# Nine small per-partition tables take 64 B instead of 256 B each, and the buffers behind them move in SBUF

## What is computed

```
qn = q / (norm(q, axis=rows) + 1e-6);  kn likewise
a  = softmax(kn^T @ qn / tau)                 # 256 x 256
x  = v @ a                                    # 6016 x 256
h  = x @ w_in1;  g = h - tanh(h);  x2 = g @ w_out1
h2 = x2 @ w_in2; g2 = where(h2 > 0, h2, exp(min(h2, 0)) - 1)
out = g2 @ w_out2
```

## Time and profile before

| | us |
|---|---|
| median of 3 runs (lowest to highest) | 1094.74 (1094.33 to 1095.83) |
| the profiled execution's own time | 1094.33 |
| its span, first to last instruction | 1092.5 |
| PE busy | 1083.3 (99%) |
| PEld busy | 907.8 (83%) |
| DVE busy | 708.0 (65%) |
| ACT busy | 536.1 (49%) |

### The profile page before, as it was taken

One profiled execution on the slowest core, in us unless ns is written; L12 is line 12 of the kernel. 1 busy time (PEld: TensorE's weight loads), 2 busy tenths in 40 slices (PEclk: granted clock), 3 DMA queues, 4 the chain that ended last, 5 costly groups with the idle time before them and its releaser, 6 DMA issues.

```text
span 1092.5 us, 14169 instructions
## 1 busy us (share of the span) xinstructions
PE 1083.3 (99%) x4908; PEld 907.8 (83%) x4908; DVE 708.0 (65%) x1139; ACT 536.1 (49%) x893; POOL 0.8 (0%) x7
## 2 busy tenths in 40 slices
PE   8999999999999999999999999999999999999998
PEld 7887888888888888888888888888888888888898
DVE  5886666666665766666666666666576666666565
ACT  6675545444444544544544544444454454444443
POOL 0000000000000000000000000000000000000000
PEclk9999999999999999999999999999999999999999
DMA  9941010110100101101011011010010010000010
GB/s 355 324 120 20 1 20 0 20 20 1 20 6 15 20 0 19 19 0 19 0 19 19 0 19 19 0 19 13 6 19 0 14 19 0 0 14 7 1 20 15
DMA packets 106237, 33.42 MB, mean 31 GB/s; under 512 B 96864, under 2 KB 101344, under 8 KB 105952
## 3 DMA queue, kind: packets, MB, share of 16 engines
q1 hardware_dynamic: 105776, 32.13, 11.7%
q10 hardware_dynamic: 432, 0.92, 0.2%
HBM read 26.87 MB, written 6.16 MB: 30 GB/s over the span
## 4 chain that ended last, share of the span: by engine, by line
PE 97%; DVE 1%; ACT 0%; DMA 0%; issue 0%; ACTq 0%
PE h_ps L375 15%; PE h_ps L377 15%; PE h_ps L376 15%; PE x_ps L375 8%; PE x_ps L376 8%; PE x_ps L377 8%; PE out_ps L375 8%; PE out_ps L376 8%; PE out_ps L377 8%; PE x_ps L383 4%; DMA q_ring<-q_dram 0%; DVE g_lo L710 0%; DVE wf_lo L740 0%; DVE w_out_lo L710 0%; DVE g L845 0%; ACT g_hi L651 0%
## 5 line engine op out<-in xcount | busy, mean ns | idle before, releaser
L710 DVE TENSOR_TENSOR g_lo<-g,g_hi 128x512 fp32r<-128x512 f32 (+1 forms) x384 | 261.4, 681 | 224.9 <-ACT g_hi L651 116.5
L651 ACT ACTIVATE g_hi<-g 128x512 fp32r<-128x512 f32 (+1 forms) x192 | 119.5, 622 | 205.5 <-DVE g L845 205.1
L637 ACT ACTIVATE g_hi<-g 128x512 fp32r<-128x512 f32 (+1 forms) x192 | 119.7, 624 | 131.7 <-PE x_ps L377 70.3
L644 ACT ACTIVATE g<-h_ps 128x512 f32<-128x512 f32 (+1 forms) x192 | 113.0, 588 | 137.2 <-PE h_ps L377 136.3
L826 DVE TENSOR_TENSOR g<-h_ps,g 128x512 f32<-128x512 f32 (+1 forms) x192 | 129.6, 675 | 30.2 <-ACT g L630 30.1
L375 PE MATMUL x_ps<-g_hi,w_out_hi 128*128 128x512 f32 (+1 forms) x384 | 148.1, 386 | 0.2 <-DVE g_lo L710 0.2
L377 PE MATMUL h_ps<-x_hi,w_in_lo 128*128 128x512 f32 (+1 forms) x384 | 148.2, 386 | 0.0
L377 PE MATMUL h_ps<-vT_hi,wf_lo 128*128 128x512 f32 (+1 forms) x384 | 148.1, 386 | 0.0
L375 PE MATMUL h_ps<-x_hi,w_in_hi 128*128 128x512 f32 (+1 forms) x384 | 148.0, 385 | 0.1
L375 PE MATMUL h_ps<-vT_hi,wf_hi 128*128 128x512 f32 (+1 forms) x384 | 148.0, 385 | 0.1
L376 PE MATMUL h_ps<-x_lo,w_in_hi 128*128 128x512 f32 (+1 forms) x384 | 147.9, 385 | 0.0
(11 more groups left out here) (105 smaller groups left out, 1091.1 us busy)
## 6 DMA issues: line engine op xcount, KB each, us to landing
v_blocks<-v_dram SPq DMA_DIRECT2D x88, 64.0 KB, 2.2
out_dram<-out_sb SPq DMA_DIRECT2D x88, 64.0 KB, 1.8
k_ring<-k_dram SPq DMA_DIRECT2D x9, 512.0 KB, 10.0
q_ring<-q_dram SPq DMA_DIRECT2D x9, 512.0 KB, 10.8
stage_a<-moe_w_in_dram SPq DMA_DIRECT2D x4, 512.0 KB, 8.3
stage_b<-moe_w_out_dram SPq DMA_DIRECT2D x1, 2048.0 KB, 8.7
w_in_raw<-moe_w_in_dram SPq DMA_DIRECT2D x1, 2048.0 KB, 10.8
stage_a<-moe_w_out_dram SPq DMA_DIRECT2D x1, 2048.0 KB, 8.6
```

What stands on the lines that cost most here:

```text
L637: nc.scalar.activation(g1_hi[i % 2][:, 0:n], g1[i % 2][:, 0:n], ACT.Copy).then_inc(g1_rounded, 1)
L644: nc.scalar.activation(g2[i % 2][:, 0:n], h2_ps[i % 2][:, 0:n], ACT.Exp).then_inc(exp2_ready, 1)
L651: nc.scalar.activation(g2_hi[i % 2][:, 0:n], g2[i % 2][:, 0:n], ACT.Copy).then_inc(g2_rounded, 1)
L710: return nc.vector.tensor_tensor(lo, x, hi.bitcast(F32), ALU.subtract)
```

## The change

One constant is changed:

```diff
 BLOCK = 32
-ALIGNED = 64
+ALIGNED = 16
 V_SLOT = 7
```

## The result

| | before | after |
|---|---|---|
| median of the timed runs, us | 1095.1 (4 runs, 1094.33 to 1095.83) | 1103.82 (4 runs, 1103.22 to 1104.62) |
| span of the profiled execution, us | 1092.5 | 1102.7 |
| PE busy / DVE busy / ACT busy, us | 1083.3 / 708.0 / 536.1 | 1093.3 / 708.2 / 536.2 |

The ratio is 1.0081, with a 95% interval from 1.0062 to 1.0098: the smaller tables make the kernel 0.8% slower, 8.7 us. The forecast was no change, 1094.8 us, in a range from 1093.2 to 1098.0.

The account below looks back on a forecast made before the run. TensorE's matmul count times spacing was taken as the bound. Matmuls 0, VectorE and ScalarE 0 and first chunk 0.1 us on 1094.33 gave 1094.4, put on the median 1094.8 us; range 1093.2 to 1098.0.

Parts of the forecast that it names:

- What bounds the kernel: Whole span: number of TensorE matmuls times their spacing sets the end; shorter waits can return at most 5.9 us.
- The tables themselves, VectorE and ScalarE: Nine small tables, and VectorE and ScalarE work on moved operands: 0 taken for each; 0.5 us kept for the tables' range.
- Matmuls on moved operands: Groups C and D (block 2), 2352 matmuls reading buffers 1728 B lower: 0 taken, bounds 0 and 7.05 ns each, 16.6 us.
- the rival: C and D matmuls pay for starting at an odd multiple of 64 B: 2.2 to 16.6 us slower; chance 0.11.
- The sign of being wrong: Forecast is wrong if C or D is spaced over 1 ns more than unmoved A and B (block 1).
- The 16-byte lines of the Trainium skill: SBUF is read in 16-byte lines; offsets 128 and 192 need the same lines for a contiguous operand, so price 0.
- Transfers: DMA into and out of moved buffers: only the first pair exposed, 0.1 us taken, ends 0 and 1.3 us.
- The DMA rule of the Trainium skill: Descriptors not starting at a multiple of 256 B pay extra; ring rows 1.5% or 2.9% more, first pair some 0.04 us later.
- The range: Whole kernel: 1093.2 to 1098.0 us, taking the forecast's own range and the lower half of the matmul case's small end.

Follow-up runs that it names:

- e5: Kernel before with 64 B unused in front of everything, so every large buffer starts at 192 modulo 256; 1095.3 us, ratio 1.0000.
- e11: Kernel before, padded so both blocks' streamed operands start at 192 and weights at 128 modulo 256; 1102.7, 1103.4, 1116.3, 1117.0 us, ratio 1.0155.
- e13: Kernel before with 64 B unused in front and 192 B behind the tables: block 1 at 192, block 2 at 128; 1103.4 us, ratio 1.0073.
- e9: Kernel before with 128 B unused in front of everything, so every large buffer starts at a multiple of 256; 1095.1 us, ratio 1.0000.
- e12: Changed kernel with 192 B unused behind the small tables: all large buffers at 128, those behind 1536 B lower than before; 1095.0 us, ratio 0.9998.
- e15: Kernel before, padded so only the rings and block 2's weights start at 192, all streamed operands at 128; 1113.2 us, ratio 1.0161.
- e3: Changed kernel with 64 B unused behind w_in2_lo: block 2's streamed operands at 0, its weights still at 192; 1105.2 us, ratio 1.0093.
- e4: Kernel before with 64 B unused behind w_in2_lo: block 2's streamed operands at 192, its weights at 128; 1110.1 us, ratio 1.0136.

## Why the prediction was wrong, step by step

- **What bounds the kernel: right.** TensorE's count times spacing set the end before and sets it now; no wait grew by more than 0.1 us. (The spacing was read as 225.7 ns from a count that takes in overlaps at the edges; the start times give 226.7. That 1 ns is as large as the 0.93 ns at which a loss was to be seen, but it doesn't move the forecast.)
- **The tables themselves, VectorE and ScalarE: right.** Busy times are within 0.2 us, and rounding takes 632 and 631 ns against 633 and 632.
- **Matmuls on moved operands: this step failed.** It took 0 from bounds of 0 and 7.05 ns for each of 2352 matmuls, and bounded 0.93 ns as the point from which it would be seen. The measured 8.7 us would be 3.7 ns on each, inside the bounds, and the rival's loss was up to 16.6 us. In place of 0 the runs showed 53 ns for each round of 24 matmuls, 8.3 us from the first C to the last B. What was wrong is the reason for the low end. Equal groups at addresses from 16512 to 218496 were read as "the place does not matter"; but all of them had the same offset against 256 B, and that was the one thing that the change touched. A control that shares the property under test excludes nothing.
- **The rival was wrong in its mechanism.** I had priced an odd start as a cost of its own, with A and B as the undisturbed control. e5 has only odd starts and costs nothing, and A, with unmoved operands, slowed down by up to 6.3 ns at its second position, and makes 14 of the 53 ns. The sign of being wrong, C or D spaced by over 1 ns more than A and B, did come: 230.3 and 230.0 ns against 228.9 and 226.5. What would have been the price of unequal offsets between neighbours was in no row.
- **The 16-byte lines of the Trainium skill** (SBUF — State Buffer, "Door 1: The DMA port swizzle") gave 0 for this step, since all starts are multiples of 16. The measurement decides: 8.7 us for a pair of offsets that are both multiples of 64. The rule speaks of successive accesses to a line; it says nothing of two operands beside each other.
- **Transfers: right in size.** The first wait is 4.8 us against 4.7 and later chunks cause none. The DMA rule of the Trainium skill (DMA: Bandwidth & Descriptors, "How a descriptor splits into AXI transactions") agrees with the traces off the path: the stores out of out_sb land in 1.9 us in all seven profiles with out_sb at offset 160 or 192, and in 1.8 us in all ten with it at 0 or 128, that of the earlier trace rows among them. That holds for reads out of SBUF alone: the v loads take 2.2 to 2.3 us in every profile, also in e5, e11 and e13, where `v_blocks` starts at 192.
- **The range** ended at 1098.0 by taking in only the lower half of the small end of a case with no idle time to cover it. With a bound of 16.6 us, an unseen condition and no cover, that case deserved more than 0.11.

What stays open is the mechanism within TensorE's reads: why 64 B apart the loss goes on for three positions of A and through C into D, though both of block 2's operands have the same offset there, while 128 B apart it stays at the change; why the shorter matmuls show none; and what sets the two levels of e11. That unequal offsets among TensorE's operands cost the time is shown by e5, e9 and e12 (equal offsets, no loss) against e13 and e15; that streams and weights of different offsets are enough is shown by e11. Whether the loss at a change of block is this same meeting, of the last stream with the next group's weights, or the change itself, is not separated.

## What to carry to other kernels

Where TensorE is the bound, let all its operands, streamed and weights, start at the same offset modulo 256 B (shown here for matmuls of 512 columns); a small tensor of odd size between two large ones can cost 1% without any instruction changing. Pad small tables together to a multiple of 256 B (here 768 B in all, e12, instead of 2304 B). Before trusting that an address does not matter, check that the rows compared differ in the property that the edit changes.

## What the runs showed of the hardware that was not expected

- Offsets of operands against each other matter, absolute ones do not: all at 0, 128 or 192 gives 1095.0 to 1095.3 us; a difference of 32, 64 or 128 B between the blocks gives 10.1, 8.0 to 9.2 and 4.2 us more; a difference of 64 B between the streams and the weights of block 2 gives 10.5 us (e3), 15.4 us (e4) and 17.8 us (e15).
- A difference of 256 B is none: before, block 1 starts at 128 modulo 512 and block 2 at 384, with no loss.
- TensorE's first 7 to 14 scores records are issued at the lower clock, every 427 ns instead of 216 ns, while the views print 1.00; this alone moves a profiled span by up to 1.6 us.
- Matmuls of 384 and 256 columns show no loss at offsets that cost those of 512 columns up to 10 ns.
